# High parts of made weights: from GpSimd's queue to fixed places of ScalarE's; attention transposes one product earlier

## What is computed

```python
scores = scale * np.matmul(q_c, k_c.transpose(0, 1, 2, 4, 3))   # per chunk of 64 tokens
attn = exp(scores - max) / (sum + 1e-09)
x = np.matmul(attn, v_c)             # then [4608 tokens, 512]
h = x @ w_in                         # [4608, 2048]
g = np.maximum(h, 0.0) + alpha * np.minimum(h, 0.0)
y = g @ w_out                        # [4608, 512]
h = y @ w_in2
g = h - np.tanh(h)
out = g @ w_out2
```

## Time and profile before

| | |
|---|---|
| median of 3 runs | 1568.79 us (1568.77 to 1569.25) |
| profiled execution | 1570.4 us, its span 1568.6 us |
| busy in the span: PE, weight loads | 97%, 95% |
| DVE, ACT, POOL | 77%, 46%, 36% |
| granted TensorE clock, mean | 0.996 |
| bytes moved by DMA | 463.36 MB, 295 GB/s |
| GpSimd's busy time | ends after some 910 us |

### The profile page before, as it was taken

How to read it: one execution, slowest core, us unless ns; L and a number is a source line. 1 busy time by engine, 2 the same in 40 slices (tenths; PEclk the granted TensorE clock), 3 DMA queues, 4 the chain that set the end, 5 groups by cost and what they waited for, 6 DMA issues and landing times.

```text
span 1568.6 us, 30311 instructions
## 1 busy us (share of the span) xinstructions
PE 1517.5 (97%) x11622; PEld 1484.0 (95%) x11622; DVE 1211.1 (77%) x1555; ACT 723.2 (46%) x1379; POOL 570.6 (36%) x754
## 2 busy tenths in 40 slices
PE   5999999999999999999988999999999999999998
PEld 5999999999899999999978999999999999999998
DVE  7988676868977997896897786686687687687685
ACT  5566454546446555653343254244244244244243
POOL 4973347878645436555788710000000000000000
PEclk8999999999999999999999999999999999999999
DMA  7695986889999899989999978868768868867765
GB/s 256 243 328 195 353 325 243 291 302 358 320 354 354 297 347 346 329 285 359 368 318 335 360 282 280 302 248 274 296 250 271 306 244 274 311 244 263 274 250 180
DMA packets 105053, 463.36 MB, mean 295 GB/s; under 512 B 12496, under 2 KB 35024, under 8 KB 62672
## 3 DMA queue, kind: packets, MB, share of 16 engines
q1 hardware_dynamic: 87344, 404.27, 72.0%
q0 software_dynamic: 17280, 56.64, 9.9%
q10 hardware_dynamic: 288, 0.52, 0.1%
HBM read 375.40 MB, written 85.98 MB: 294 GB/s over the span
## 4 chain that ended last, share of the span: by engine, by line
PE 70%; DVE 16%; DMA 5%; issue 5%; ACT 2%; POOL 1%; SPq 0%; DVEq 0%; ACTq 0%
PE banks L665 12%; PE banks L667 11%; PE banks L666 11%; PE banks L744 8%; PE banks L746 8%; PE banks L745 8%; DVE go_lo L1275 6%; DVE g_full L1297 3%; DMA ring<-w_split 2%; PE banks L694 2%; DVE g_full L1253 2%; PE banks L696 2%; PE banks L695 2%; PE banks L737 2%; PE banks L739 1%
## 5 line engine op out<-in xcount | busy, mean ns | idle before, releaser
L665 PE MATMUL banks<-xo_hi,ring 128*128 128x384 f32 x1344 | 455.7, 339 | 7.2 <-DMA ring<-w_split 3.3
L667 PE MATMUL banks<-xo_hi,ring 128*128 128x384 f32 x1344 | 450.5, 335 | 1.1 <-issue 1.1
L666 PE MATMUL banks<-xo_lo,ring 128*128 128x384 f32 x1344 | 450.3, 335 | 0.0
L1275 DVE TENSOR_TENSOR go_lo<-g_full,go_hi 128x768 fp32r<-128x768 f32 x344 | 364.7, 1062 | 77.6 <-ACT go_hi L955 75.1
L955 ACT CAST go_hi<-g_full 128x768 fp32r<-128x768 f32 x344 | 286.0, 836 | 253.5 <-PE banks L746 105.8
L744 PE MATMUL banks<-ring,go_hi 128*128 128x256 f32 x1008 | 285.5, 283 | 0.0
L745 PE MATMUL banks<-ring,go_hi 128*128 128x256 f32 x1008 | 285.2, 283 | 0.0
L746 PE MATMUL banks<-ring,go_lo 128*128 128x256 f32 x1008 | 285.2, 283 | 0.0
L665 PEld LDWEIGHTS banks<-xo_hi,ring 128*128 128x128 f32 x1344 | 253.1, 188 | 14.1 <-issue 7.5
L667 PEld LDWEIGHTS banks<-xo_hi,ring 128*128 128x128 f32 x1344 | 253.0, 188 | 1.5 <-issue 1.5
L666 PEld LDWEIGHTS banks<-xo_lo,ring 128*128 128x128 f32 x1344 | 253.3, 188 | 0.0
(11 more groups left out here) (135 smaller groups left out, 2304.5 us busy)
## 6 DMA issues: line engine op xcount, KB each, us to landing
ring<-w_split SPq DMA_DIRECT2D x302, 1024.0 KB, 6.5
w_split<-sums POOLq DMA_DIRECT2D x112, 256.0 KB, 6.6
w_split<-ring SPq DMA_DIRECT2D x22, 1024.0 KB, 5.3
qkv<-in_chunks SPq DMA_DIRECT2D x60, 256.0 KB, 7.9
w_split<-made_first POOLq DMA_DIRECT2D x56, 256.0 KB, 6.8
raw<-in_weights POOLq DMA_DIRECT2D x48, 256.0 KB, 7.7
x_raw<-y_between SPq DMA_DIRECT2D x6, 1536.0 KB, 9.7
out<-stage SPq DMA_DIRECT2D x24, 384.0 KB, 7.5
```

The source lines that it names most:

```text
L665: nc.tensor.matmul(h, hi, xo_hi[:, o, k, :], start=fresh and k == 0, stop=False, skip_group_check=not fresh)
L666: nc.tensor.matmul(h, hi, xo_lo[:, o, k, :], start=False, stop=False, skip_group_check=not fresh)
L667: last = nc.tensor.matmul(h, lo, xo_hi[:, o, k, :], start=False, stop=k == 1, skip_group_check=not fresh)
L1275: nc.vector.tensor_tensor(go_lo[:, slot, :, :], g_of(s, n), go_hi[:, slot, :, :], ALU.subtract).then_inc(glo_ready, 1)
```

## The change

1. GpSimd no longer copies the high parts, and no longer waits for TensorE's place: `pace` is gone. ScalarE copies them in `high_beside`, called at fixed places of its order: in the first half of runs 1 to 6 once after `act_c11` and once after `act_rest` of each pair (twice in run 5), and 2 (run 6: 3) times at the half's end; in the second half of run 1 once in each of units 2 to 25; in the second halves of runs 2 to 5 ten times. Per run: 40, 26, 26, 26, 33, 17. The wait for the store of block k-3 moves to ScalarE with the copy, and so does a wait for GpSimd's sums (`made_step`) or the chunk's load.
2. In GpSimd's queue each sum stands ahead of the low part that it used to follow.
3. In runs 1 to 4 TensorE does the transposes of a pair of units ahead of product 7 instead of behind it.
4. At the end of run 0, SP issues the first group of run 1 ahead of the loads of q, k and v.

```diff
-def pace(k):
-    for s, count, first, tenths in ((1, 14, 2, 37), (1, 25, FIRST_BLOCKS, 12), (2, 19, 2, 26), (2, 8, 60, 60), (3, 16, 2, 32), (3, 8, 60, 60),
-                                    (4, 16, 2, 32), (4, 8, 60, 60), (5, 20, 2, 26), (5, 20, 58, 25), (6, 14, 2, 32)):
...
@@ keep_block
                 here = made_places[k % 3]
-                pool.wait_ge(block_done, done(*pace(k)))
-                if k >= 3:
-                    pool.wait_ge(made_stored[k % 3], 16 * (k // 3))
-                nc.gpsimd.tensor_copy(here[:, 0, :], src).then_inc(made_high, 1)
                 pool.wait_ge(made_high, k + 1)
@@ GpSimd, per chunk
+                nc.gpsimd.tensor_tensor(a21, a21, a22, ALU.add).then_inc(made_step, 1)
                 keep_block(k, a11)
-                nc.gpsimd.tensor_tensor(a21, a21, a22, ALU.add).then_inc(made_step, 1)
                 pool.wait_ge(made_step, 4 * c + 1)
+                nc.gpsimd.tensor_tensor(a11, a21, a11, ALU.subtract).then_inc(made_step, 1)
                 keep_block(k + 1, a21)
-                nc.gpsimd.tensor_tensor(a11, a21, a11, ALU.subtract).then_inc(made_step, 1)
...
@@ TensorE, phase_a
                 for p in range(2, PAIRS):
-                    for u in late_pair(s, p - 2):
-                        transpose_attn(u)
                     product(s, 6, p)
...
                     product(s, 2, p)
+                    for u in late_pair(s, p - 1):
+                        transpose_attn(u)
                     product(s, 7, p)
@@ ScalarE
+            def high_beside(count):
+                for k in range(made["beside"], min(made["beside"] + count, len(MADE))):
+                    c, i = divmod(k, 7)
+                    a11, a12, a21, a22 = made_quarters(c)
+                    if i in (1, 2, 4, 5):
+                        act.wait_ge(made_step, 4 * c + {1: 1, 2: 2, 4: 3, 5: 4}[i])
+                    else:
+                        act.wait_ge(raw2_in[c % 2], 32 * (c // 2 + 1))
+                    if k >= 3:
+                        act.wait_ge(made_stored[k % 3], 16 * (k // 3))
+                    nc.scalar.copy(made_places[k % 3][:, 0, :], (a11, a21, a11, a12, a21, a12, a22)[i]).then_inc(made_high, 1)
+                    made["beside"] = k + 1
@@ ScalarE, phase_a, pair p
                     act_c11(s, p - 1)
+                    if 0 < s <= SUPER:
+                        high_beside(1)
...
                         act_rest(s, p - 1)
                     high_parts(s, base(p) + 5 + AHEAD)
+                    if 0 < s <= SUPER:
+                        high_beside(1 if s != SUPER - 1 else 2)
                 act_c11(s, PAIRS - 1)
+                if 0 < s <= SUPER:
+                    high_beside(2 if s < SUPER else 3)
@@ ScalarE, plain_phase_b, unit n
                         high_g(s, n + 2)
+                    if s and 2 <= n < 26:
+                        high_beside(1)
@@ ScalarE, phase_b, step n
                         high_g(s, n + 2)
+                    if s < SUPER and n in (1, 4, 7, 10, 13, 15, 17, 20, 25, 27):
+                        high_beside(1)
@@ SP, make_groups
                 store_y(s, 0)
+                load_group(group_base(s + 1))
                 load_ahead(s + 2, 0)
```

More of the change, by code:

```diff
@@ L169 @@
         for layer, second in ((0, True), (1, False), (1, True)) for p in range(PAIRS) for i in MADE_ORDER]
-def pace(k):
-    for s, count, first, tenths in ((1, 14, 2, 37), (1, 25, FIRST_BLOCKS, 12), (2, 19, 2, 26), (2, 8, 60, 60), (3, 16, 2, 32), (3, 8, 60, 60),
-                                    (4, 16, 2, 32), (4, 8, 60, 60), (5, 20, 2, 26), (5, 20, 58, 25), (6, 14, 2, 32)):
-        if k < count:
-            return s, first + tenths * k // 10
-        k -= count
-    raise ValueError(k)
 def dram_group(layer, q, plainly):
@@ L413, in raw_of, with made_quarters @@
             return sum_of(name, p)
+        def made_quarters(c):
+            q = [[raw[:, c % 2, i, m * 256:(m + 1) * 256] for m in range(2)] for i in range(2)]
+            return (q[0][0], q[0][1], q[1][0], q[1][1]) if c // PAIRS == 1 else (q[0][0], q[1][0], q[0][1], q[1][1])
         def block_of(s, j):
@@ L531, in _ @@
                 pool.wait_ge(raw2_in[c % 2], 32 * (c // 2 + 1))
-                quarter = [[raw[:, c % 2, i, m * 256:(m + 1) * 256] for m in range(2)] for i in range(2)]
-                a11, a22 = quarter[0][0], quarter[1][1]
-                a12, a21 = (quarter[0][1], quarter[1][0]) if c // PAIRS == 1 else (quarter[1][0], quarter[0][1])
+                a11, a12, a21, a22 = made_quarters(c)
+                nc.gpsimd.tensor_tensor(a21, a21, a22, ALU.add).then_inc(made_step, 1)
                 keep_block(k, a11)
-                nc.gpsimd.tensor_tensor(a21, a21, a22, ALU.add).then_inc(made_step, 1)
                 pool.wait_ge(made_step, 4 * c + 1)
+                nc.gpsimd.tensor_tensor(a11, a21, a11, ALU.subtract).then_inc(made_step, 1)
                 keep_block(k + 1, a21)
-                nc.gpsimd.tensor_tensor(a11, a21, a11, ALU.subtract).then_inc(made_step, 1)
                 pool.wait_ge(made_step, 4 * c + 2)
+                nc.gpsimd.tensor_tensor(a21, a22, a11, ALU.subtract).then_inc(made_step, 1)
                 keep_block(k + 2, a11)
                 keep_block(k + 3, a12)
-                nc.gpsimd.tensor_tensor(a21, a22, a11, ALU.subtract).then_inc(made_step, 1)
+                nc.gpsimd.tensor_tensor(a12, a12, a11, ALU.subtract).then_inc(made_step, 1)
                 pool.wait_ge(made_step, 4 * c + 3)
                 keep_block(k + 4, a21)
-                nc.gpsimd.tensor_tensor(a12, a12, a11, ALU.subtract).then_inc(made_step, 1)
                 pool.wait_ge(made_step, 4 * c + 4)
@@ L830, in _ @@
         def _(act):
-            made = {0: 0}
+            made = {0: 0, "beside": 0}
             def high_part(j):
@@ L1595, in make_groups @@
                 store_y(s, 0)
+                load_group(group_base(s + 1))
                 load_ahead(s + 2, 0)
-                for group in range(group_base(s + 1), group_base(s + 1) + RING - 1):
+                for group in range(group_base(s + 1) + 1, group_base(s + 1) + RING - 1):
                     load_group(group)
```

## The result

| | before | after |
|---|---|---|
| median (lowest to highest) | 1569.0 us (1568.8 to 1571.2, 4 runs) | 1595.2 us (1594.1 to 1599.2, 4 runs) |
| profiled execution, its span | 1570.4, 1568.6 us | 1594.65, 1592.9 us |
| busy: DVE, ACT, POOL | 1211, 723, 571 us | 1209, 774, 455 us |

What follows compares the result with a forecast made beforehand. TensorE was busy nearly throughout; run 5's second half was limited by VectorE, slowed by GpSimd's SBUF work. Terms -10 + 11 + 4 + 6 + 2 - 3.5 = +9.5, less 1.5: 1568.8 + 8 = 1577 us, range 1556 to 1591.

Steps and rivals of the forecast that it cites:

- Run 5 B, -10: Run 5, second half: 10 us gained as GpSimd's work falls and stops slowing VectorE; bounds 8 and 11.
- Run 5 A, +11: Run 5, first half: 11 us lost as ScalarE's copies wait for stores to land; bounds 5 and 15.
- Run 6, +4: Run 6, entry into second half: 4 us lost, last copy's store wait delays the third step; bounds 2.5 and 5.
- Run 1 B, +6: Run 1, second half: 6 us lost, GpSimd's pace of 2.7 us a block holds ScalarE; bounds -1 and +12.
- Attention, +2: First halves of runs 1 to 4: 2 us lost, outputs wait behind ScalarE's added copies; bounds -4 and +6.
- The rest, -3.5: 3.5 us gained: 1.5 from issuing run 1's first group early, 2 in the halves of runs 2 to 4.
- Emptier queues, -1.5: Whole sum: 1.5 us taken off because longer TensorE waits leave emptier transfer queues and stores land sooner.
- the places never run out: Rival: stores land fast enough and GpSimd keeps one block per unit, so faster, 1556 us; chance 0.18.

Runs made afterwards that it cites:

- run 0: Not a follow-up run: a stretch of the kernel itself, ahead of run 1; its second half (B) took 78.9 us before the change and 77.8 after.
- best7: Changed kernel, but ScalarE copies only 20 blocks in run 5's second half, GpSimd all others; seven places from the end of run 4: 1564.2 us.
- run5_even: Changed kernel, three places, with run 5's 33 copies dealt out as 16 in its first half and 17 in its second: 1585.4 us.
- act_only: Changed kernel with the transposes and run 1's first group put back as before, leaving the copies alone: 1600.8 us, ratio 1.0195.
- tr_only: Kernel before the change with only the transposes moved ahead of product 7: 1568.8 us, ratio 0.9994.
- places7: Changed kernel with seven places instead of three for made blocks in run 1's second half and from the end of run 4 on: 1567.1 us.
- p7_behind: Changed kernel with seven places and, in runs 1 to 4, the copy behind `place_attnT` instead of ahead of it: 1569.7 us, ratio 1.0009.
- sp_only: Kernel before the change with only run 1's first group issued ahead of the eight loads: 1568.6 us, ratio 0.9986.

## Why the prediction was wrong in size

- **Run 5 B, -10:** -10.55. Right, with its mechanism: `go_lo` took 1081 ns. What the prediction didn't separate is whether fewer copies or fewer blocks do it; best7 and run5_even show that it is the blocks.
- **Run 5 A, +11:** +13.3 (in act_only, with the same code in this half, +19.3). The chain held (stores landed after 6.3 to 6.4 us by the median, and copies waited for them), and ScalarE's lateness was about what was worked out: TensorE's idle time grew by (74.0 - 64.03) - (60.7 - 60.16) = 9.4 us. The place was wrong. I had all of it in one stall ahead of the third step; it came in three: two at `copy_s1`, which stands behind a copy in the middle of the pairs, and one at the first steps. And the term had no clock in it: (3.40 + 3.95) / 2 = 3.7 us of slow matmuls. Its lower bound was also miscounted: a cycle of 7.5 us gives 11.5 - 6 x 0.75 = 7, not 5.
- **Run 6, +4:** -1.7 in A and +6.9 in B, 5.2 together. The one stall at the third step was there, 5.3 us where I had 4.0, plus 2.34 / 2 = 1.2 for the clock. The -1.7 in A need be no effect of the change: tr_only, whose code of run 6 is the old one, has it as well (60.6 us).
- **Run 1 B, +6:** +13.6. This is the step that failed, in its mechanism. I had GpSimd's pace as the limit, at 2.7 us a block. The low parts took 0.79 us, not the 1.24 of the earlier trace rows, and by my own lower bound the term would then have been -1. (The upper bound, 12, comes out as 10 when the sum is made with 2.9 us a block.) GpSimd was not the limit; it stood idle for ScalarE's copies. GpSimd in that half:

```profile
L496 POOL TENSOR_TENSOR sums<-raw,sums 128x256 fp32r<-128x256 f32 x17 | 13.3, 781 | 9.8 <-ACT sums L852 9.7
...
L496 POOL TENSOR_TENSOR made_first<-raw,made_first 128x256 fp32r<-128x256 f32 x9 | 7.2, 797 | 7.0 <-ACT made_first L852 7.0
```

  The limit was the same chain as in run 5 A. I didn't compute it here because the landing of 4.1 us before the change gives 0.4 + 0.1 + 1.24 + 0.3 + 4.1 = 6.1 us, just under three units (6.2). With no slack at all in the sum it should have carried an allowance: the landings became 5.3 and 5.9 us by the median.

```profile
w_split<-sums POOLq DMA_DIRECT2D x17, 256.0 KB, 5.3
w_split<-made_first POOLq DMA_DIRECT2D x9, 256.0 KB, 5.9
```

  The copies waited 26.1 us for these, and `places7`, which takes nothing from GpSimd's work, takes 12.0 of the 13.6 us away: what failed is the limit that I took for this half; it was the landing of block k-3, and not GpSimd's pace. A cycle of 7.5 us makes 2.5 a block and, less the 2.7 us of tolerance, 23 x (2.5 - 2.08) - 2.7 = 7 us; measured were 2.93 a block. The rest I put down to uneven landings (the longest 8.6 us), which is argued from the trace and not isolated by a run, and 5.51 / 2 = 2.8 to the clock.
- **Attention, +2:** -0.2, +0.1, +2.0, +1.5 in runs 1 A to 4 A, 3.4, each within what stretches differ by. The outputs' wait for the copied probabilities rose from 4.0 us to 13.7. My term put this down to one copy standing ahead of them; but with that copy behind them it is still 11.0 (p7_behind). The copies alone make it 13.3 (act_only) and the transposes alone 7.8 (tr_only), so the transposes were not without effect on it either. What the other 7 us come from stays open.
- **The rest, -3.5:** -0.8. Run 0 B gave 1.1 of 1.5 (in sp_only 0.5); the second halves of runs 2 to 4 gave -2.0, +0.8 and +1.5 instead of -2.
- **Emptier queues, -1.5:** stores in run 5 A did land a little sooner, but that gain was in the 9.4 us already, and in run 1 B they landed later. There was no reason for a deduction over the whole sum.

The differences to the forecast: run 1 B 7.6, run 5 A 2.3, run 6 1.2, run 5 B -0.55, attention 1.4, the rest 2.7, the deduction 1.5, in all 16.2 of the 16.3 us by which span and forecast differ. Cut the other way, 8 of them are the lower clock, which no term had. The direction was right in part by luck: run 1 B's loss was forecast from a limit that did not hold, and with the low parts as measured that term would have been -1 and the forecast near 1570, hardly a change. The rival "the places never run out" needed more places, and even with seven its 1556 us did not come: places7 took 1567, with 4.0 us more in runs 1 A to 4 A, 1.6 in run 1 B and 1.9 in run 5 A than before.

## What to carry to other kernels

A wait for a DMA that moves from an idle engine's queue into that of one which feeds TensorE has to be sized by the slow landings and not by the median alone: run 1 B had 6.1 against 6.2 us by the old median and lost 13.6, run 5 A with four places had 8.5 to 9.1 against 9.7 and lost 4.8 against seven. Count what stands behind each new instruction in its queue at every place, not at the last one alone, and give the buffers enough places before moving the wait. When a forecast contains stalls of TensorE, give it a bound in which the matmuls behind each stall of 2 us or more run at half the clock for some us: here four of the seven such stalls had that.

## What the runs showed of the hardware that I had not expected

**Stalls can lower the clock:** four spells at 0.50 behind stalls of 2.3, 3.3, 5.3 and 5.7 us, against none in the stretches of the earlier trace rows; stalls of 2.0, 2.2 and 2.7 us in the same execution had none.

**Who pays for a collision on SBUF changes.** VectorE and GpSimd in run 3 B of the changed kernel, two pairs of instructions that begin together:

```profile
567.31 1.62 DVE L1288 TENSOR_TENSOR go_lo<-g_full,go_hi 128x768 fp32r<-128x768 f32 x1
...
572.88 0.94 DVE L1200 TENSOR_TENSOR xo_lo<-x_raw,xo_hi 128x768 fp32r<-128x768 f32 x1
```

```profile
567.36 0.75 POOL L531 TENSOR_TENSOR raw<-raw 128x256 f32<-128x256 f32 x1
...
572.94 1.49 POOL L496 TENSOR_TENSOR made_first<-raw,made_first 128x256 fp32r<-128x256 f32 x1 [2.54 <-ACT made_first L852]
```

The first time VectorE's subtraction is 0.67 us longer than its 0.95, nearly GpSimd's 0.75, and GpSimd is undisturbed; the second time GpSimd's is doubled and VectorE undisturbed. "SBUF — State Buffer" of the Trainium skill, section "Terms", says that the loser of the shared ports fully blocks, and these rows agree. Which of the two loses the starts don't tell: in both pairs VectorE's begins first, by 0.05 and 0.06 us. In run 1 B of the changed kernel `go_lo` takes from 0.95 us, alone, to 2.4 and 2.6 beside two instructions of GpSimd, near 0.95 + 2 x 0.75. Over that half the price moved, from the first line (before) to the second (after):

```profile
L1275 DVE TENSOR_TENSOR go_lo<-g_full,go_hi 128x768 fp32r<-128x768 f32 x30 | 36.5, 1219 | 16.3 <-ACT go_hi L955 16.3
L1288 DVE TENSOR_TENSOR go_lo<-g_full,go_hi 128x768 fp32r<-128x768 f32 x30 | 46.1, 1562 | 21.3 <-ACT go_hi L958 21.1
```

GpSimd's low part fell from 1219 to 786 ns at the same time. Before, the two shared the price; now the one that supplies TensorE bears it.

**Late landings are not in themselves a loss.** In run 5 A of places7 the stores landed after some 12 us, twice as late as in the changed kernel, and the half took 62.6 us instead of 74.0:

```profile
w_split<-probs POOLq DMA_DIRECT2D x6, 256.0 KB, 12.1
w_split<-attnT POOLq DMA_DIRECT2D x6, 256.0 KB, 12.9
```

ScalarE still waited up to 3.3 us for a place, but TensorE was busy for 60.9 of the 62.6 us. My reading is that more places let more stores stand in the queues at a time, so that each is served later; no run isolates it.
